# The first step of a fused recurrence and two feed-forward layers: GpSimd takes the k products and the lower weight halves, loads and heads change their order

## The chip, the cores and the metric

The kernel runs on one core of a Trainium2 chip. The metric is the device time of one launch in microseconds (us); the times below are medians of several runs. Five engines work in parallel and wait for each other through semaphores: TensorE (PE in the profile), VectorE (DVE), ScalarE (ACT), GpSimd (POOL) and SyncE (SP), which here only starts transfers.

## The reference

```python
def _attn_ref(r, k, v, w, u):                       # B=4, H=8, S=768, D=48, all float32
    for t in range(S):
        kt, vt, rt, wt = (k[:, :, t], v[:, :, t], r[:, :, t], w[:, :, t])
        cur = np.einsum('bhd,bhe->bhde', u[None] * kt, vt)
        y[:, :, t] = np.einsum('bhd,bhde->bhe', rt, state + cur)
        state = wt[:, :, :, None] * state + np.einsum('bhd,bhe->bhde', kt, vt)

x = y as 3072 tokens x 384
h = x @ w_in;  x = where(h > 0, h, exp(min(h, 0)) - 1) @ w_out          # d_ff 2048
h = x @ w_in2; x = (h / (1 + exp(-1.702 h))) @ w_out2                   # d_ff 2048
```

## The kernel before

The tokens are cut into 8 steps of 384 (half a batch entry). For each step the kernel computes the recurrence of the 8 heads, and it sends the 384 tokens (one group) through the first feed-forward layer while the next step's recurrence runs beside it. After the 8 steps all groups go through the second layer. Every operand of the feed-forward matmuls is split into a high and a low half (`x_hi`, `x_lo`; `w_split` holds both halves of the weights; `g_hi`, `g_lo`), and each product is three matmuls.

The recurrence of a step is chunked. `wtree` holds running products of the decay w over 2, 4, ... 64 tokens ("tree"). In six levels k = 1 to 6, r and k are multiplied by these decays (`update_r`, `update_k`), and after each of them TensorE computes the scores of that distance (`products`); level k+1 waits for its products. `pick_diag` and `pick` take the valid scores out of the banks under a mask (COPY_PREDICATED), `assemble` copies them together, `turn` transposes k, `keys_values` multiplies it with v, `states` runs the chain over the chunks (one copy, then five times `faded = state * wchunk` and `state = faded + psum`), and `outputs` forms y from scores (`from_scores`) and states (`from_state`). Heads lie in two halves of the partitions (`a` = 0, 1) and four slots u; in the first step the slots are worked in two pairs (pair 0: u = 0, 1; pair 1: u = 2, 3), so (k, pair) names a level below, as (2,0).

Two of the 8 heads (slot u = 3) do not fit into the 384 = 3 x 128 rows of x as they come out. Their rows go through the tile `y3` and are moved by transfers of 16 rows into the gaps of `x_raw` ("gap transfers", x_raw<-y). Then `first_split` makes x_hi on ScalarE and x_lo on VectorE, and `up(0, 0, 0)` starts the feed-forward part.

In the first step nothing else is there for TensorE, so its time is bare. The first layer's 16 weight tiles (384 KB each) arrive in it and in the next: `w1_high` on ScalarE makes the high half, `w1_low` on VectorE the lower one, GpSimd starts the transfers (`load`).

From step 1 on TensorE's queue is written out by hand in `step`. `unit(f)` is `up` of tile f+2 (nine matmuls into `hidden`) and `down` of tile f; levels, turns and outputs of the recurrence stand between the units. ScalarE applies the exponential, VectorE `gated`, ScalarE `gate_hi`, VectorE `gate_lo`. The argument s shifts the recurrence behind the units: with s = 1 one whole unit is done before level 1, and `split` of the next group comes after tile 15, with s = 0 after tile 14. Step 1 runs with s = 1, the six steps behind it with s = 0. `near(i+1)`, the first scores of the next step, closes each step.

## Time and profile before

| | |
|---|---|
| median of 3 runs | 1003.53 us (1003.37 to 1005.42) |
| profiled execution: its own time | 1003.23 us |
| its span | 1001.2 us |
| PE busy | 948.9 us, 95% |
| DVE, ACT, POOL busy | 545.1, 456.2, 54.9 us |
| mean granted PE clock | 0.986 of full speed |

The profiled execution took 1003.23 us, of which the span from the first to the last instruction is 1001.2 us. Rows of the timeline and of the chain begin with the start and the length in us from the span's start. A bracket such as [3.17 <-DVE x_lo L730] gives the idle time of the engine just before the row and what ended it. A granted clock of 1.00 is full speed.

### The profile page before, as it was taken

What the parts mean: (1) busy time and instruction counts of PE and PEld (TensorE: products, weight loads), DVE (VectorE), ACT (ScalarE), POOL (GpSimd) and SP (SyncE); (2) the same over time, 40 slices, a digit from 0 to 9 for tenths busy, and PEclk for the clock granted to TensorE, in tenths of its full rate; (3) what the DMA queues carried; (4) which work ended last, traced back from release to release, by engine and by line L of the source; (5) the groups of instructions that cost most, each with busy time, mean ns of one, the idle gap of its engine ahead of it and who ended that gap; (6) DMA issues with size and microseconds to landing.
All of it is one profiled execution on the core that took longest, in us unless ns stands there. A gap on an engine that the chain in (4) does not pass through costs nothing.

```text
span 1001.2 us, 27033 instructions
## 1 busy us (share of the span) xinstructions
PE 948.9 (95%) x11872; PEld 920.2 (92%) x11872; DVE 545.1 (54%) x903; ACT 456.2 (46%) x861; POOL 54.9 (5%) x64
## 2 busy tenths in 40 slices
PE   3659989999999999999999999999999999999998
PEld 3559989989889899999999999999999999999998
DVE  6758757476585686675764444343434343434333
ACT  3344834635536537456455674333333333333332
POOL 3010000000000000000000352000000000000000
PEclk9879999999999999999999999999999999999999
DMA  7242130231211211302102630000000000000000
GB/s 203 73 124 68 41 94 11 49 80 26 56 51 26 55 50 26 102 4 55 49 2 86 252 111 1 1 24 1 24 0 24 0 24 0 24 1 24 1 24 24
DMA packets 15413, 47.29 MB, mean 47 GB/s; under 512 B 2864, under 2 KB 6832, under 8 KB 15312
## 3 DMA queue, kind: packets, MB, share of 16 engines
q1 hardware_dynamic: 12688, 38.19, 13.8%
q0 software_dynamic: 2016, 6.86, 2.3%
q8 instruction: 87, 1.43, 0.6%
q10 hardware_dynamic: 608, 0.70, 0.3%
q14 instruction: 14, 0.11, 0.0%
HBM read 35.71 MB, written 8.85 MB: 45 GB/s over the span
## 4 chain that ended last, share of the span: by engine, by line
PE 91%; issue 3%; DVE 3%; DMA 1%; ACT 1%; POOL 0%; DVEq 0%; ACTq 0%; SPq 0%; POOLq 0%
PE psum L1119 40%; PE psum L1132 39%; PE psum L971 4%; PE psum L1071 2%; PE psum L1032 1%; PE psum L934 1%; PE psum L1066 1%; PE psum L980 1%; PE psum L997 1%; DMA x_raw<-y 1%; DMA arena<-r_channels_dram 1%; DVE arena L641 0%; DVE x_lo L730 0%; DVE blocks L695 0%; ACT x_hi L419 0%
## 5 line engine op out<-in xcount | busy, mean ns | idle before, releaser
L1119 PE MATMUL psum<-x_hi,w_split 128*128 128x384 f32 x1536 | 395.0, 338 | 0.0
L1132 PE MATMUL psum<-g_hi,w_split 128*128 128x384 f32 x1536 | 392.9, 337 | 0.0
L1119 PEld LDWEIGHTS psum<-x_hi,w_split 128*128 128x128 f32 x1536 | 281.3, 189 | 1.4 <-issue 1.4
L1132 PEld LDWEIGHTS psum<-g_hi,w_split 128*128 128x128 f32 x1536 | 278.6, 189 | 0.1
L1119 PE MATMUL psum<-x_lo,w_split 128*128 128x384 f32 x768 | 264.3, 344 | 12.1 <-DVE x_lo L725 5.3
L1132 PE MATMUL psum<-g_lo,w_split 128*128 128x384 f32 x768 | 262.3, 342 | 0.8 <-issue 0.7
L444 ACT ACTIVATE g_hi<-gate 128x384 fp32r<-128x384 f32 x256 | 134.5, 525 | 175.8 <-DVE gate L743 93.5
L748 DVE TENSOR_TENSOR g_lo<-gate,g_hi 128x384 fp32r<-128x384 f32 x256 | 142.7, 557 | 118.9 <-ACT g_hi L444 118.9
L741 DVE TENSOR_TENSOR gate<-expo,psum 128x384 f32<-128x384 f32 x128 | 70.8, 553 | 162.9 <-ACT expo L440 162.9
L1119 PEld LDWEIGHTS psum<-x_lo,w_split 128*128 128x128 f32 x768 | 144.6, 188 | 14.5 <-DVE w_split L769 5.5
L1132 PEld LDWEIGHTS psum<-g_lo,w_split 128*128 128x128 f32 x768 | 145.0, 189 | 3.8 <-issue 1.6
L440 ACT ACTIVATE expo<-psum 128x384 f32<-128x384 f32 x128 | 63.0, 492 | 172.9 <-PE psum L1119 172.9
L743 DVE SCALAR_TENSOR_TENSOR gate<-expo,psum 128x384 f32<-128x384 f32 x128 | 70.9, 554 | 128.4 <-ACT expo L435 128.3
L433 ACT ACTIVATE expo<-psum 128x384 f32<-128x384 f32 x128 | 62.6, 489 | 146.0 <-PE psum L1119 145.7
L635 DVE TENSOR_TENSOR arena<-arena 128x1536 f32<-128x1536 f32 (+1 forms) x54 | 85.1, 1575 | 9.8 <-PE psum L971 8.9
L435 ACT ACTIVATE expo<-expo 128x384 f32<-128x384 f32 x128 | 67.2, 525 | 4.0
L971 PEld LDWEIGHTS psum<-arena 128*32 128x32 f32 (+1 forms) x3840 | 41.9, 112 | 21.3 <-issue 16.7
L971 PE MATMUL psum<-arena 128*32 128x32 f32 (+1 forms) x3840 | 47.5, 204 | 12.8 <-issue 9.1
L641 DVE TENSOR_TENSOR arena<-arena 128x768 f32<-128x768 f32 (+1 forms) x54 | 46.5, 862 | 0.0
L328 POOL DMA_DIRECT2D x_raw<-y x21 | 10.1, 486 | 425.4 <-DVE y L720 425.4
L695 DVE COPY_PREDICATED blocks<-masks,psum 128x384 f32<-128x384 int32 x40 | 30.3, 757 | 2.0 <-DVE blocks L695 1.6
L388 ACT ACTIVATE blocks<-blocks 32x768 f32<-32x768 f32 x32 | 26.9, 840 | 1.2 <-DVE blocks L695 0.6
(75 smaller groups left out, 448.0 us busy)
## 6 DMA issues: line engine op xcount, KB each, us to landing
v_sb<-v_tokens_dram SPq DMA_DIRECT2D x8, 576.0 KB, 5.9
arena<-w_channels_dram SPq DMA_DIRECT2D x14, 288.0 KB, 4.8
arena<-k_channels_dram SPq DMA_DIRECT2D x14, 288.0 KB, 4.4
arena<-r_channels_dram SPq DMA_DIRECT2D x14, 288.0 KB, 4.8
x_scratch<-x_sb SPq DMA_DIRECT2D x7, 576.0 KB, 3.2
arena<-x_scratch SPq DMA_DIRECT2D x1, 4032.0 KB, 12.9
staging<-weights_dram POOLq DMA_DIRECT2D x10, 384.0 KB, 3.6
blocks<-weights_dram SPq DMA_DIRECT2D x9, 384.0 KB, 3.9
```

What stands on the lines that cost most here:

```text
L433: act.activation(expo[:, f % 2, :], hidden(f), ACT.Relu, scale=-1.0).then_inc(neg_done, 1)
L435: act.activation(expo[:, f % 2, :], expo[:, f % 2, :], ACT.Exp, scale=-1.0).then_inc(exp_done, 1)
L440: act.activation(expo[:, f % 2, :], hidden(f), ACT.Sigmoid, scale=1.702).then_inc(exp_done, 1)
L444: act.activation(g_hi[:, f % 4, :], gate[:, f % 2, :], ACT.Copy).then_inc(hi_done, 1)
L635: return dve.tensor_tensor(z, z, by, ALU.mult)
L641: return dve.tensor_tensor(z, z, d[:, :, 1:2].to_broadcast([P, d.shape[1], h]), ALU.mult)
L741: dve.tensor_tensor(gate[:, f % 2, :], expo[:, f % 2, :], hidden(f), ALU.mult).then_inc(gate_done, 1)
L743: dve.scalar_tensor_tensor(out=gate[:, f % 2, :], in0=expo[:, f % 2, :], scalar=-1.0, in1=hidden(f), op0=ALU.add, op1=ALU.max).then_inc(ga ...
L748: dve.tensor_tensor(g_lo[:, f % 4, :], gate[:, f % 2, :], g_hi[:, f % 4, :].bitcast(F32), ALU.subtract).then_inc(lo_done, 1)
L971: mm = pe.matmul(bank[32 * j:32 * j + n, at:at + 32].rearrange("p (a b h) -> p a b h", a=2, h=h), kk[:, u, o:o + n], r[:, :, u, o:o + 32]. ...
L1119: mm = pe.matmul(hidden(f), w_tile(f, lo, m * P), xx, start=n == 0, stop=n == 3 * KT - 1)
L1132: mm = pe.matmul(acc(to, m), w_tile(f, lo, (KT + m) * P), gg, start=f == 0 and n == 0, stop=f == NF - 1 and n == 2)
```

## The change

In the first step:

- SP loads r of a pair ahead of w. ScalarE issues k of pair 1 only after its table load. SP, not GpSimd, starts the first five weight tiles, right behind the first loads.
- VectorE multiplies only r (`grow_r_pair`). GpSimd multiplies k (`grow_k_pair`) and makes the whole tree of pair 1 (`tree_second`). The products wait for both.
- All 16 `w1_low` run on GpSimd. Loads of later tiles stand between them in its queue.
- The clearing of `blocks` moves from GpSimd to VectorE.
- The outputs of slot u = 3 have two banks of their own (`FIRST[6 + c % 2]`) and are computed first (`first_outputs`); `y3` is copied from them by ScalarE and VectorE at once, and the gap transfers (four on SP, two on ScalarE) start before the other outputs are done. The rest of x_raw is copied in pieces of 48 rows, which leave the gaps alone.
- The tree of step 1 comes after `first_split` on VectorE.

In step 1, s goes from 1 to 0, and the weight tiles' high halves take other places in ScalarE's queue (8 and 9 behind tiles 0 and 1, 10 to 15 behind tiles 2 to 7).

```diff
+                def tree_second(m):
+                    us = slice(2, 4)
...
+                    pool.tensor_tensor(dst[:, us], s4[:, :, :, 0], s4[:, :, :, 1], ALU.mult).then_inc(tree_done, 1)
+                def grow_k_pair(k, pair):
...
+                    pool.wait_ge(lev_first[pair], k)
+                    pool.wait_ge(w_first[pair], 32)
...
+                    pool.tensor_tensor(z, z, d[:, :, 1:2].to_broadcast([P, d.shape[1], h]), ALU.mult).then_inc(updk_first[pair], 1)
...
+                def w1_low(f):
+                    pool.wait_ge(whi_done, f + 1)
+                    at = 2 * f * WF
+                    pool.tensor_tensor(w_split[:, at + WF:at + 2 * WF], w1_raw[w1_place(f)],
+                                       w_split[:, at:at + WF].bitcast(F32), ALU.subtract).then_inc(wlo_done, 1)
+                grow_k_pair(1, 0)
+                for m in range(6):
+                    tree_second(m)
+                grow_k_pair(2, 0)
+                grow_k_pair(1, 1)
+                for k in range(3, 7):
+                    grow_k_pair(k, 0)
+                    grow_k_pair(k - 1, 1)
+                grow_k_pair(6, 1)
+                for f in range(NF):
+                    w1_low(f)
+                    if f < 3:
+                        pool.wait_ge(wlo_done, f + 1)
+                        load(f + NW1)
+                    elif 5 <= f < NF - 3:
+                        pool.wait_ge(wlo_done, f + 1)
+                        load(f + 3)
...
+                def first_outputs():
...
+                    for c in (0, 2, 4):
+                        for a in range(2):
+                            from_scores(c, U - 1, a)
+                            mm = from_scores(c + 1, U - 1, a)
+                    mm.then_inc(y3_first, 1)
...
+                    pe.wait_ge(state_done, N_STATE[0])
+                    pe.wait_ge(y3_first, 1)
+                    for c in range(1, NC):
+                        for a in range(2):
+                            mm = from_state(c, U - 1, a)
+                    mm.then_inc(y3_first, 1)
...
-                outputs(0, 0, 0)
+                first_outputs()
                 up(0, 0, 0)
                 near(1)
                 up(0, 0, 1)
-                step(0, 1, 1, 0, 0, s=1)
+                step(0, 1, 1, 0, 0)
```

GpSimd's queue, from its clearing of `arena` on, before:

```order
L317 MEMSET arena 128x768 x4
L318 MEMSET blocks 128x2304
L321 DMA staging<-weights_dram 128x768 x2
L321 DMA x_sb<-weights_dram 128x768
L321 DMA expo<-weights_dram 128x768
L321 DMA gate<-weights_dram 128x768
L321 DMA staging<-weights_dram 128x768 x2
L321 DMA x_sb<-weights_dram 128x768
```

And the same place in the changed kernel (L366 multiplies k, L352 is the tree of pair 1):

```order
L339 MEMSET arena 128x768 x4
L366 ISA
L366 TENSOR_TENSOR arena<-arena 128x384
L352 TENSOR_TENSOR arena<-arena 128x384
L352 TENSOR_TENSOR arena<-arena 128x192
L352 TENSOR_TENSOR arena<-arena 128x96
L352 TENSOR_TENSOR arena<-arena 128x48
L352 TENSOR_TENSOR arena<-arena 128x24
L352 TENSOR_TENSOR wchunk<-arena 128x12
L366 TENSOR_TENSOR arena<-arena 128x192x2
L366 TENSOR_TENSOR arena<-arena 128x384
```

The transfers are gone from the start of this queue; k of (1,0), the six tree products, then k of (2,0) and (1,1) stand there, ten more k products follow, and behind them the 16 lower halves (L382).

VectorE's queue at the end of the first step's levels, before (L676 and L695 are picks, L635 is r, L641 is k, L769 is `w1_low`, L704 to L712 are the states):

```order
L676 COPY_PREDICATED blocks<-masks,psum 128x384 x2
L635 TENSOR_TENSOR arena<-arena 128x2x12x32
L641 TENSOR_TENSOR arena<-arena 128x12x32
L695 COPY_PREDICATED blocks<-masks,psum 128x384
L695 COPY_PREDICATED blocks<-masks,psum 128x192x2
L695 COPY_PREDICATED blocks<-masks,psum 128x96x4
L695 COPY_PREDICATED blocks<-masks,psum 128x48x8
L695 COPY_PREDICATED blocks<-masks,psum 128x24x16
L769 TENSOR_TENSOR w_split<-staging,w_split 128x768 x2
L704 COPY state<-psum 128x192
L709 TENSOR_TENSOR faded<-state,wchunk 128x192
L712 TENSOR_TENSOR state<-faded,psum 128x192
```

And in the changed kernel (L747 and L766 are picks, L707 is r):

```order
L747 COPY_PREDICATED blocks<-masks,psum 128x384 x2
L707 TENSOR_TENSOR arena<-arena 128x2x24x16
L766 COPY_PREDICATED blocks<-masks,psum 128x384
L707 TENSOR_TENSOR arena<-arena 128x2x12x32
L766 COPY_PREDICATED blocks<-masks,psum 128x192x2
L766 COPY_PREDICATED blocks<-masks,psum 128x96x4
L766 COPY_PREDICATED blocks<-masks,psum 128x48x8
L766 COPY_PREDICATED blocks<-masks,psum 128x24x16
L775 COPY state<-psum 128x192
L780 TENSOR_TENSOR faded<-state,wchunk 128x192
L783 TENSOR_TENSOR state<-faded,psum 128x192
```

The first pick now stands ahead of the last r product, the k products and the two lower halves are gone, and the states follow the picks directly.

TensorE's queue around level 1 of step 1, before: the last third of `up` of tile 3, the level, and the start of `down` of tile 1.

```order
L1119 MATMUL psum<-x_lo,w_split 128x384
L1119 MATMUL psum<-x_hi,w_split 128x384 x2
L971 MATMUL psum<-arena 32x32 [waits pick_done,upd_done]
L971 MATMUL psum<-arena 32x32 x47
L1132 MATMUL psum<-g_lo,w_split 128x384 [waits lo_done]
L1132 MATMUL psum<-g_hi,w_split 128x384 x2
```

In the changed kernel the same rows are the last third of `up` of tile 2, the level, and the start of `down` of tile 0.

```order
L1230 MATMUL psum<-x_lo,w_split 128x384
L1230 MATMUL psum<-x_hi,w_split 128x384 x2
L1030 MATMUL psum<-arena 32x32 [waits pick_done,upd_done]
L1030 MATMUL psum<-arena 32x32 x47
L1243 MATMUL psum<-g_lo,w_split 128x384 [waits lo_done]
L1243 MATMUL psum<-g_hi,w_split 128x384 x2
```

The level moved ahead by `down` of tile 0 and `up` of tile 3, 18 matmuls, which now follow it.

## Rows read from the trace of the kernel before

**Rows 1.** The page, part 2: busy tenths of TensorE in 40 slices of 25 us

```profile
PE   3659989999999999999999999999999999999998
```

**Rows 2.** Windows: span; length; busy (count) PE, PEld, DVE, ACT, POOL; clock; DMA; GB/s

```profile
65.00:137.40 72.40, 63.86 (x989) 60.37 (x987) 51.22 (x78) 41.11 (x76) 4.68 (x9) 0.93 0.29 75
142.90:205.40 62.50, 61.17 (x989) 57.92 (x987) 41.73 (x69) 34.11 (x66) 1.43 (x3) 1.00 0.21 52
80.00:127.80 47.80, 47.27 (x825) 44.98 (x824) 37.09 (x60) 30.41 (x57) 4.15 (x8) 1.00 0.22 58
127.80:137.40 9.60, 6.43 (x30) 5.71 (x28) 3.55 (x5) 4.13 (x7) 0.00 (x0) 0.82 0.57 130
```

**Rows 3.** Timeline, 6 to 13 us: the first waits for loads

```profile
6.07 1.10 ACT L364 ACTIVATE arena<-arena,ucol 128x384 f32<-128x384 f32 x2
7.04 1.70 DVE L622 TENSOR_TENSOR arena<-arena 128x384 f32<-128x384 f32 x5 [1.87 <-DMA arena<-w_channels_dram]
...
9.65 1.51 PE L934 MATMUL psum<-arena 128*32 128x64 f32 x48 [9.65 <-DMA arena<-r_channels_dram]
...
11.65 1.25 POOL L321 DMA_DIRECT2D staging<-weights_dram  x2 [6.18 <-DMA arena<-w_channels_dram]
11.85 0.96 DVE L635 TENSOR_TENSOR arena<-arena 128x768 f32<-128x768 f32 x1 [2.90 <-PE psum L971]
```

**Rows 4.** Timeline, 15 to 46 us, VectorE: levels, picks, lower halves, states

```profile
15.92 0.55 DVE L641 TENSOR_TENSOR arena<-arena 128x384 f32<-128x384 f32 x1
...
28.77 0.96 DVE L635 TENSOR_TENSOR arena<-arena 128x768 f32<-128x768 f32 x1 [0.26 <-PE psum L980]
...
38.67 0.59 DVE L695 COPY_PREDICATED blocks<-masks,psum 128x384 f32<-128x384 int32 x1 [0.26 <-DVE blocks L695]
39.14 1.83 DVE L769 TENSOR_TENSOR w_split<-staging,w_split 128x768 fp32r<-128x768 f32 x2
40.87 0.36 DVE L704 COPY state<-psum 128x192 f32<-128x192 f32 x1
...
44.85 0.36 DVE L712 TENSOR_TENSOR state<-faded,psum 128x192 f32<-128x192 f32 x1
```

**Rows 5.** The chain that ended last, from the outputs to the first `up`

```profile
49.51 0.56 DVE x_raw L719
...
50.99 2.50 DMA x_raw<-y
53.51 0.53 ACT x_hi L414
...
54.77 3.22 PE psum L1119 x9
```

**Rows 6.** The same chain around level 1 of step 1

```profile
69.65 2.09 issue
71.74 1.14 PE psum L971 x66
72.87 2.75 issue
```

**Rows 7.** Timeline, TensorE: first matmul behind the split of group 1 and of group 2

```profile
132.50 0.44 PE L1119 MATMUL psum<-x_lo,w_split 128*128 128x384 f32 x1 [3.17 <-DVE x_lo L730]
...
202.08 0.44 PE L1119 MATMUL psum<-x_lo,w_split 128*128 128x384 f32 x1 [0.54 <-DVE x_lo L730]
```

**Rows 8.** Timeline, 569 to 577 us: GpSimd and VectorE side by side

```profile
569.52 1.85 POOL L349 TENSOR_TENSOR w_split<-blocks,w_split 128x768 fp32r<-128x768 f32 x1 [1.28 <-ACT w_split L463]
572.93 1.36 DVE L735 TENSOR_TENSOR x_lo<-arena,x_hi 128x1152 fp32r<-128x1152 f32 x1 [0.50 <-ACT x_hi L427]
573.71 2.29 POOL L349 TENSOR_TENSOR w_split<-blocks,w_split 128x768 fp32r<-128x768 f32 x1 [2.35 <-ACT w_split L463]
575.74 0.67 DVE L748 TENSOR_TENSOR g_lo<-gate,g_hi 128x384 fp32r<-128x384 f32 x1 [0.59 <-ACT g_hi L444]
```

**Rows 9.** The page, part 5: g_lo in all groups (busy, mean ns, idle before)

```profile
L748 DVE TENSOR_TENSOR g_lo<-gate,g_hi 128x384 fp32r<-128x384 f32 x256 | 142.7, 557 | 118.9 <-ACT g_hi L444 118.9
```

**Rows 10.** Timeline, SP: two gap transfers of the first step

```profile
50.34 1.23 SPq L243 DMA_DIRECT2D x_raw<-y  x2
```

More of the change, by code:

```diff
@@ L148, in build @@
         level_open, pick_open, gap_open = sem("level_open"), sem("pick_open"), sem("gap_open")
-        w1_in = [sem(f"w1_in{q}") for q in range(NW1)]
+        w1_in = [sem(f"w1_in{q}") for q in range(3)]
         w2_in = [sem(f"w2_in{q}") for q in range(NW2)]
@@ L195, in tokens, with y3_first_view, x_first_rows @@
             return chunks[:, z, 0:2] if z < 2 else chunks[:, :, 2]
+        def y3_first_view(par):
+            return (y3[:].rearrange("p m (c two t) -> p two c m t", c=NB, two=2)[:, par],
+                    FIRST[6 + par][:, 0:NB * CH].rearrange("p (c m t) -> p c m t", c=NB, m=1))
+        def x_first_rows(z, a):
+            rows = slice(64 * a, 64 * a + D)
+            return tokens(x_raw[:], z)[rows], of_heads(0, z, 0, KT)[rows]
         def of_heads(i, z, u0, u1):
@@ L278, in _ @@
                                      r_dram[0, a][:, cols]).then_inc(r_first[pair], 16)
+                    sp.wait_ge(cleared_w, pair + 1)
+                    first_pair(arena[:, 3 * UT:4 * UT], w_dram, pair, w_first)
                 sp.dma_start(v_sb[:].rearrange("p c u a e -> p (c u a e)"), v_dram[0]).then_inc(v_in, 16)
                 sp.dma_start(ident[:, :], ident_dram).then_inc(ident_in, 16)
+                for f in range(NW1):
+                    sp.dma_start(w1_raw[f], weights1[f]).then_inc(w1_first[f], 16)
                 step(0)
@@ L542, in _, with load_k @@
                 act.dma_start(ucol[:, :], ucol_dram).then_inc(ucol_in, 16)
-                for pair in range(2):
+                def load_k(pair):
                     act.wait_ge(cleared_k, pair + 1)
@@ L556, in _ @@
                     w1_high(f)
-                for z in range(3):
-                    kt_copy(0, z)
                 act.wait_ge(cleared_b, 1)
@@ L576, in _ @@
                 act.wait_ge(wlo_done, NW1)
-                for f in range(2):
-                    whole(0, f)
+                whole(0, 0)
                 w1_high(8)
-                step(1, 0, 0, s=1)
+                whole(0, 1)
+                w1_high(9)
+                step(1, 0, 0)
                 with act.Fori(1, B - 1) as b:
@@ L786, in step @@
                     grow_k(i, 2)
-                    lower(8)
                     pick(i, 1)
@@ L794, in step @@
                     gate_lo(g, 4 + s)
-                    lower(9)
                     pick(i, 4)
@@ L808, in step @@
                     gate_lo(g, 7 + s)
-                    lower(12)
                     pick(i, 16)
@@ L1209, in _ @@
                 up(0, 0, 1)
-                step(0, 1, 1, 0, 0, s=1)
+                step(0, 1, 1, 0, 0)
                 with pe.Fori(1, B - 1) as b:
```

218 lines of the change are left out of this document (134 added, 84 removed).

## The prediction, made before the change was run

> **What bounds the kernel now.** I read the busy slices first [rows 1]: TensorE is at 8 or 9 tenths from the fourth slice on, and at 3 to 6 tenths in the first three. The change touches nothing behind step 1, so only the first 140 us can give anything. Then the windows [rows 2]. From the `up` of tile 2 to the first scores of the next step (`near`), step 1 takes 72.4 us and step 2 takes 62.5 us, for the same 989 recorded matmuls. So the first step is bare waiting, and step 1 carries 9.9 us that its successor doesn't. Between 80 and 127.8 us TensorE is busy for 47.27 of 47.8 us: work taken off other engines there is worth nothing. The chain shows the rest: r's load holds the first scores until 9.65 [rows 3], VectorE runs the levels and picks until 39.26 and the states until 45.21 [rows 4], the gap transfers hold x_hi until 53.51 [rows 5], and TensorE waits 2.09 and 2.75 us around level 1 [rows 6] and 3.17 us behind the split [rows 7]. (Each of these ends is the row's start and length together.)
>
> **What GpSimd and VectorE do to each other.** This decides the case, and the trace has two encounters [rows 8]. A GpSimd product of 768 columns takes 1.85 us alone. One that starts at 573.71, while VectorE's x_lo (two inputs in SBUF) runs until 574.29, takes 2.29 us and ends at 576.00, which is 1.71 us after x_lo's end. VectorE's g_lo, started at 575.74 under it, takes 0.67 us instead of the usual 0.56 [rows 9], and ends 0.41 us after 576.00. Both fit one reading: of two such instructions only one reads at a time, and about 0.15 us of each (1.85 less 1.71, 0.56 less 0.41) lies outside that hold. I take it. A GpSimd product then holds VectorE's two-input products for 1.71 us at 768 columns, or 2.23 ns a column. VectorE's own holds are 0.96 - 0.15 = 0.81 us for r and less for the others.
>
> The Trainium skill says the same, and it is what speaks against this change: "SBUF — State Buffer", section "SBUF: two separate sides", has the port pair that the two share as an exclusive lock for the whole instruction, between a GpSimd operation and a VectorE operation with two SBUF inputs. By that rule the sum is the one below; by free sharing it would be the first rival's.
>
> **The change, part by part.**
>
> *Start.* r of pair 0 moves from fourth to second in the line of loads, w from second to third. w arrived second at 7.04 [rows 3], so r should be there by then, and the two k scalings (1.10 us [rows 3]) end near 7.2, as k is in by 6.07 or earlier. First scores at about 7.2 instead of 9.65: the first r product at 9.4 instead of 11.85, -2.4 us.
>
> *Tree on GpSimd.* w of pair 1 is now last of six loads. Fifth of six it freed GpSimd at 11.65 [rows 3]; I put it at 12.5. The six tree products have 756 columns: 756 x 2.23 ns + 6 x 0.15 = 2.6 us, with waits on its own semaphore 2.9. Two r products of VectorE (0.8 each) fall into it, and half a microsecond is lost ahead of it. k of (2,0) has 384 columns: 384 x 2.23 ns + 0.15 = 1.0 us. It stands behind the tree and ends near 12.5 + 0.6 + 2.9 + 0.8 + 1.0 = 17.8 us. Before it ended at 16.47 [rows 4]. The head start is gone: +1.3 us.
>
> *Levels.* VectorE needed 0.96 + 0.55 us for a pair of r and k, less overlap. Now r holds 0.81 and k 0.86 us, in turn: 1.67 a pair, 3.3 a level. Before, from k of (2,0) at 15.92 to r of (6,0) at 28.77 [rows 4], four levels took 12.85 us, 3.2 each, since VectorE also waited for TensorE. The pace is the same, and with one round trip less at the end r of (6,0) starts near 28.8 again. No gain from the split.
>
> *Picks.* From r of (6,0) to the last pick took 10.5 us (28.77 to 39.26 [rows 4]). Three k products go (some 0.4 us each), the first pick moves into a wait for TensorE, but r and k of (6,1) queue for the hold. I take 9.3: picks end at 38.1, -1.2 us.
>
> *States.* They no longer stand behind two lower halves (1.83 us [rows 4]) and start near 38.4 instead of 40.87. But GpSimd, which ends its last k near 35.5, now runs lower halves one behind the other, 1.86 us each, and five of the chain's eleven links (`faded`) read two SBUF tiles. Before the chain took 4.3 us (40.87 to 45.21). If every `faded` meets a lower half it takes 11.5, if the transfers that GpSimd issues between its products let most through, 7.3. I take 9.2, as three such gaps exist for five links: the states end at 47.6 instead of 45.21, +2.4 us.
>
> *y and the gaps.* From the states' end to the first `up` took 54.77 - 45.21 = 9.6 us [rows 4, 5]. The gap transfers now start about 1 us after the states: three issues of 0.6 us on SP [rows 10] ahead of the fourth, and its landing of 2.5 us [rows 5], make 5.3 with it. The rest of y takes 4.4 us on TensorE (45.21 to 49.51 before, and one wait more), and then come three copies of 0.56 [rows 5] on VectorE instead of the transfers: 6.1 us. So x_hi starts at +6.1 instead of +8.3 (53.51 - 45.21), -2.2. Then 1.26 us to the first matmul as before. The lower half of tile 7 is started just then, since its high half stands right ahead of x_hi on ScalarE, and holds the first x_lo: +1.0 us. First `up` at 47.6 + 6.1 + 1.26 + 1.0 = 56.0 against 54.77: +1.2 us in all for the first step.
>
> *Step 1.* Before, 82.6 us lie between the first `up` (54.77) and `near(2)` (137.4), 10.2 of them ahead of tile 2's `up` (at 65.0), 72.4 behind. With s = 0 the latter part is arranged as in step 2, which takes 62.5 [rows 2]. TensorE still waits for level 1's k product. Two lower halves (1.9 us) leave VectorE's line ahead of it, a hold of 1.71 us may come into it, and the level now stands one `down` and one `up` nearer; the tree fits into the time of `near`. I keep 2.1 us [rows 6]. What goes is the 3.17 us behind the split, as step 2's 0.54 shows [rows 7], with the low clock behind it (granted 0.82 in that stretch, 1.00 in step 2's [rows 2]), some 1.5 us. The 2.75 us inside level 1 [rows 6] wait for nothing that the profile shows; its place moves by 18 matmuls, so it may go or stay. I put clock after the wait and this at 1.7 us. The lower halves leave VectorE (8 x 0.95 us), but each holds it for 1.71 us; between levels 2 and 3 VectorE has no slack: +0.8 us. Sum: 10.2 + 62.5 + 2.1 + 1.7 + 0.8 = 77.3 against 82.6, -5.3 us.
>
> *Total.* +1.2 - 5.3 = -4.1 us. Against the profiled execution's own 1003.23 us (0.3 below the median of the runs shown) that is 999.1 us. Most of it is the step from s = 1 to 0, not the work given to GpSimd.
>
> **Bounds.** The hold: between nothing and every link met, the states end between 43 and 50. The k product on GpSimd: not below its share of columns, 0.93 us, nor above a whole 1.85. The wait inside level 1: 0 to 2.75. w of pair 1: 11.65 to 13.5.
>
> **Rivals.**
>
> *No hold, the engines share.* Two encounters may be chance. Then the tree ends at 15.5, a level takes 3.0 us (TensorE's own round trip and its own pauses), the states and the scores' matmuls end at 42.3, and the first `up` comes 7.4 us later, at 49.7 instead of 54.77 (6.1 + 1.26 as above) and level 1 isn't held either: -5.1 - 5.3 - 1.6 = -12.0, 991.2 us (1.6: level 1's product and levels 2 and 3 without a hold). Chance 0.13.
>
> *The k product is dearer on GpSimd, and it ends slower.* Its inputs are strided and one is broadcast; no row shows such a form. Eleven of them stand in one line. At 1.0 us they keep pace; each tenth more costs 1.1 us. From 1.37 us on the 4.1 us are gone, and at 1.55 the kernel is 2 us slower: 999.1 + 11 x 0.55 = 1005.2. For it speaks that the 1.85 us is the only price known, against it that a column costs VectorE the same in both forms. Chance 0.11.
>
> *The lower halves hold VectorE back in step 1.* VectorE is busy for 37.1 of 47.8 us there [rows 2]; 8 x 0.95 go and up to 8 x 1.71 us of hold come. If the levels come late by 1 us each, four of them, the 4.1 us are lost: 1003.2, no change. Against it: TensorE's queue has one unit of slack for all but the levels, and a lower half starts behind g_lo, when VectorE's next product has begun. Chance 0.13.
>
> **How the numbers follow.** The forecast, 999.1, has 0.63; its own range is 996 to 1002.5, from the states' end (45.7 to 50) and the wait inside level 1. 0.2% is 2 us, about what a measurement can tell: faster is below 1001.5, slower above 1005.5. Faster: 0.56 of the forecast's 0.63 and all of the first rival's 0.13, 0.69. Slower: 0.08 from the second and 0.02 from the third, 0.10. Same: 0.21. The range, 992 to 1004, leaves out most of the first rival and the slower part of the second, about 2 in 10.
>
> **What would show it.** The k products on GpSimd at 1.0 us alone and near 1.8 when r runs; `faded` at up to 2 us each instead of 0.36; k of (2,0) ended near 17.8; the first `up` near 56; step 1's wait behind the split down to under 1 us at full clock. It is wrong if `faded` stays at 0.36 beside lower halves (then it is 991), if k products take over 1.4 us, or if TensorE waits more than a microsecond in all between 80 and 125 us.

## The result and the profile after

The changed kernel takes 1011.18 us (median of 6 runs, 1008.21 to 1012.43), the kernel before beside it 1004.93 (6 runs, 1003.37 to 1006.34): ratio 1.0064, 95% interval 1.0048 to 1.0080. It is 0.6% slower. The prediction had 999.1 us, a range of 992 to 1004 and a chance of 0.10 for slower. The profiled execution took 1011.4 us (span 1009.4).

The page's busy tenths, TensorE's to set beside [rows 1]: its second slice is at 5, where it was at 6, and GpSimd is busy in the first five. TensorE's granted clock (third row) is lowest in the second slice, where it waits most.

```profile
PE   3559999999999899999999999999999999999998
...
POOL 6836100000000000000000262000000000000000
PEclk8569999999999999999999999999999999999999
```

Timeline of the start, of VectorE and GpSimd, beside [rows 3]:

```profile
9.14 0.56 DVE L694 TENSOR_TENSOR arena<-arena 128x384 f32<-128x384 f32 x1 [1.52 <-DMA arena<-w_channels_dram]
9.73 1.21 DVE L694 TENSOR_TENSOR arena<-arena 128x192 f32<-128x192 f32 x1
10.87 0.94 DVE L707 TENSOR_TENSOR arena<-arena 128x768 f32<-128x768 f32 x1
```
```profile
9.26 1.47 POOL L366 TENSOR_TENSOR arena<-arena 128x384 f32<-128x384 f32 x1 [5.74 <-PE psum L1030]
12.34 0.83 POOL L352 TENSOR_TENSOR arena<-arena 128x384 f32<-128x384 f32 x1 [1.61 <-DMA arena<-w_channels_dram]
...
15.75 1.01 POOL L366 TENSOR_TENSOR arena<-arena 128x384 f32<-128x384 f32 x1
```

The first scores now start at 6.98, but w of pair 0, behind k and r, comes at 9.14 instead of 7.04, and the second tree product (9.73, 1.21 us for 0.36) stands behind GpSimd's k of (1,0). So the first r product comes at 10.87 (11.85 before), not at 9.4. k of (2,0) on GpSimd ends at 16.76, but TensorE, which stopped at 14.43 among the first products of pair 1, goes on with them and with level 2 only at 17.43:

```profile
17.43 0.82 PE L1030 MATMUL psum<-arena 128*32 128x32 f32 x67 [3.00 <-issue]
```

The 3.00 us ahead of them wait for nothing that the profile shows.

The states start at 41.19, later than the last pick (it ends at 39.99). The chain that ended last shows what they waited for:

```profile
35.24 1.62 POOL arena L366
...
36.91 1.54 PE psum L1056 x6
...
39.18 1.99 PE psum L1091 x64
...
41.19 0.37 DVE state L775
```

The last k product, k of (6,1), runs on GpSimd until 36.86; the turns (L1056) and keys times values (L1091) follow, and then the first copy of the states. Before, VectorE ended that product at 34.56. So it is GpSimd's line, not VectorE's picks, that lets the states start here.

The timeline of VectorE and GpSimd while the states run, to set beside the last lines of [rows 4]. The states are a chain of eleven operations, here called links. L780 is the link `faded`, a product of two SBUF tiles; L783 adds from PSUM; L369 issues a weight transfer, L382 is a lower half of a weight tile:

```profile
41.85 0.56 POOL L369 DMA_DIRECT2D staging<-weights_dram  x1 [0.31 <-POOL w_split L382]
...
42.37 2.10 DVE L780 TENSOR_TENSOR faded<-state,wchunk 128x192 f32<-128x192 f32 x1
42.43 1.81 POOL L382 TENSOR_TENSOR w_split<-x_sb,w_split 128x768 fp32r<-128x768 f32 x1
...
44.51 0.35 DVE L783 TENSOR_TENSOR state<-faded,psum 128x192 f32<-128x192 f32 x1
44.54 0.56 POOL L369 DMA_DIRECT2D x_sb<-weights_dram  x1 [0.30 <-POOL w_split L382]
44.89 5.78 DVE L780 TENSOR_TENSOR faded<-state,wchunk 128x192 f32<-128x192 f32 x1
45.12 1.82 POOL L382 TENSOR_TENSOR w_split<-expo,w_split 128x768 fp32r<-128x768 f32 x1
...
46.91 1.79 POOL L382 TENSOR_TENSOR w_split<-gate,w_split 128x768 fp32r<-128x768 f32 x1
48.66 1.79 POOL L382 TENSOR_TENSOR w_split<-staging,w_split 128x768 fp32r<-128x768 f32 x1
50.71 0.35 DVE L783 TENSOR_TENSOR state<-faded,psum 128x192 f32<-128x192 f32 x1
50.75 0.56 POOL L369 DMA_DIRECT2D staging<-weights_dram  x1 [0.30 <-POOL w_split L382]
51.16 2.20 DVE L780 TENSOR_TENSOR faded<-state,wchunk 128x192 f32<-128x192 f32 x1
```

A link that takes 0.36 us alone takes 5.78: it starts at 44.89, during the issue at 44.54 and before the half of 45.12, and ends after the third half, at 50.67. The additions from PSUM stay at 0.35. From 41.19 to 54.53 the chain takes 13.3 us, where it took 4.3.

The chain that ended last, beside [rows 5]: x_hi, x_lo, the first `up`.

```profile
60.44 0.53 ACT x_hi L474
60.99 1.51 DVE x_lo L796
...
62.63 3.22 PE psum L1230 x9
```

The first `up` is 7.9 us later than before (54.77). Step 1 gives most of it back: `near(2)` starts at 138.84 against 137.38. But another 6.6 us go behind it, between `near(2)` and `near(7)`: 347.8 us (138.84 to 486.66) against 341.3 (137.38 to 478.64). Together these are 8.0 of the 8.2 us between the two profiled executions. The starts of `near` of the steps 2 to 7 are from TensorE's timeline at its line; from one to the next (steps 2 to 6) it takes 67.9, 71.1, 72.3, 69.1, 67.4 us after, and 68.0, 68.5, 70.0, 67.3, 67.4 before.

### The profile page after: what moved, and what is told of

Its sections match the earlier page's. It is cut to its first block, busy times and chain, and to the rows that moved or that the text cites. A ratio compares the mean times of both kernels' runs of the same rounds, so it can differ in the third digit from the quotient of the medians.

```text
span 1009.4 us, 27078 instructions
## 1 busy us (share of the span) xinstructions
PE 951.9 (94%) x11872; PEld 922.3 (91%) x11872; DVE 550.2 (55%) x872; ACT 456.9 (45%) x861; POOL 104.4 (10%) x90
## 4 chain that ended last, share of the span: by engine, by line
PE 91%; issue 3%; DVE 2%; DMA 1%; POOL 1%; ACT 0%; SPq 0%; DVEq 0%; POOLq 0%; ACTq 0%
PE psum L1230 40%; PE psum L1243 39%; PE psum L1030 3%; PE psum L1130 2%; PE psum L1091 1%; PE psum L1039 1%; PE psum L1125 1%; DVE faded L780 1%; PE psum L1056 1%; PE psum L991 1%; DMA x_raw<-y 1%; DMA arena<-w_channels_dram 1%; POOL arena L366 0%; PE psum L1179 0%; POOL arena L352 0%
## 5 line engine op out<-in xcount | busy, mean ns | idle before, releaser
L819 DVE TENSOR_TENSOR g_lo<-gate,g_hi 128x384 fp32r<-128x384 f32 x256 | 147.7, 577 | 117.8 <-ACT g_hi L504 117.7
L707 DVE TENSOR_TENSOR arena<-arena 128x1536 f32<-128x1536 f32 (+1 forms) x54 | 89.4, 1658 | 12.2 <-PE psum L1030 10.7
L495 ACT ACTIVATE expo<-expo 128x384 f32<-128x384 f32 x128 | 67.2, 525 | 4.0
L713 DVE TENSOR_TENSOR arena<-arena 128x768 f32<-128x768 f32 x42 | 41.3, 984 | 0.0
L766 DVE COPY_PREDICATED blocks<-masks,psum 128x384 f32<-128x384 int32 x40 | 30.3, 757 | 2.2 <-DVE blocks L766 1.8
```

Source lines behind the costliest of these rows:

```text
L495: act.activation(expo[:, f % 2, :], expo[:, f % 2, :], ACT.Exp, scale=-1.0).then_inc(exp_done, 1)
L707: return dve.tensor_tensor(z, z, by, ALU.mult)
L713: return dve.tensor_tensor(z, z, d[:, :, 1:2].to_broadcast([P, d.shape[1], h]), ALU.mult)
L819: dve.tensor_tensor(g_lo[:, f % 4, :], gate[:, f % 2, :], g_hi[:, f % 4, :].bitcast(F32), ALU.subtract).then_inc(lo_done, 1)
```

## The experiments

Fifteen kernels ran; ratios are to the kernel before on the same chip. "First `up`" is the start of the first `up` matmul. A "half" is a lower or higher half of a weight tile. Times inside a kernel are from its one profiled execution.

**e1_s0: the kernel before with the step order s = 0 alone.**

```diff
-                step(0, 1, 1, 0, 0, s=1)
+                step(0, 1, 1, 0, 0)
```


> The kernel before with only step 1's s changed from 1 to 0 (and the six high halves placed accordingly). The first step is as before. My account of the change: from the first up to near(2) it takes 77 us instead of 82.6, because the 3.17 us wait behind the split and the low clock after it go, so 5 us less: 998 to 1000. Rival: the gain is given back behind step 1, in the loop, as in the changed kernel, whose near(2) came only 1.4 us later than before's but whose near(7) came 8.1 us later: then near(2) comes 5 us earlier and the end 0 to 2 us earlier.

Measured: 1000.51 us, ratio 0.9954 (0.9939 to 0.9969). First `up` at 53.3, `near(2)` at 131.2: 77.9 us between them, for 82.6 before and 77.3 predicted. The gain between them, 4.7 us, is near the 5.3 predicted for this part of the change, and the step order alone beats both kernels. The rival falls: `near(2)` to `near(7)` takes 341.5 us, as before. The first `up` is 1.5 us earlier than before (54.8) though nothing ahead of it changed, and 1.2 us earlier (53.6) in e2 below: by so much two executions of the same first step differ, and a smaller difference in one start shows nothing by itself.

**e2_pad8: the kernel before with eight empty instructions at the start of TensorE's program.** There TensorE waits for its loads anyway. The changed kernel's part ahead of the loop has eight instructions more too, 1375 for 1367.

```diff
+                for _ in range(8):
+                    pe.sem_inc(level_open, 1)
                 pe.wait_ge(cleared_p, 3)
```


> The kernel before with eight empty semaphore increments at the start of TensorE's queue, where it waits for the first loads. The changed kernel has eight instructions more in front of the loop than before has (1375 against 1367). Theory A, the place of the loop's code decides its pauses: near(2) comes as before, and near(2) to near(7) takes 346 to 348 us instead of 341.2, the whole 4 to 6 us longer. Theory B, the place does nothing: within 0.5 us of before everywhere, and the 6.7 us of the changed kernel behind step 1 have another cause.

Measured: 1008.34 us, ratio 1.0038 (1.0017 to 1.0060). The steps take 67.6, 70.8, 70.3, 69.1, 67.4 us: as in the changed kernel, the second loses 2.3 us and the fourth 1.8. `near(2)` comes at 138.3, 0.9 late, and from there to `near(7)` it takes 345.2 us, 3.9 more than before (theory A had 346 to 348 and stands; B falls). Eight more instructions ahead of the loop cost time in it, without any work changed.

**e3_late_low: the changed kernel with GpSimd's halves held until the states are done.**

```diff
                 grow_k_pair(6, 1)
+                pool.wait_ge(state_done, N_STATE[0])
```


> The changed kernel with GpSimd's lower halves held back until the states are done. Theory, the hold: the eleven links of the states take 4.3 us instead of 13.3, so near 45.5 instead of 54.5, the first up comes 8 to 9 us earlier, at 54 to 55 (some 1 us of hold by the first lower halves may come back), and near(2) 6 to 9 us earlier: 1003 to 1005. Rival: the states are slow for another reason (TensorE's own matmuls or the banks), and they still take over 10 us; or the first up then waits for the lower half of tile 0, which starts at 45.5 and ends at 47.4, which is early enough.

Measured: 1010.7 us, ratio 1.0054 (1.0037 to 1.0071). The states take 4.3 us again (40.79 to 45.14): the halves alone stretched them. But the load of tile 5 now waits for half 0, ScalarE waited 7.11 us for it in front of its copy of y3, and the first `up` came at 59.8, not at 54 to 55: the total misses the 1003 to 1005 expected.

**e4_probe: GpSimd's products measured behind the end of the kernel before.**


> The kernel before with a probe behind its end (the output is untouched). GpSimd: three plain products of 384 columns, three in the form of the k product (h = 1, 4, 32), then four of 768 columns back to back beside six VectorE products of 192 columns with two SBUF inputs, then four of 768 beside six VectorE sums with one input in SBUF and one in PSUM. My price: 1.0 us for each 384-column product in every form. Rival: the broadcast form is dearer, 1.4 us or more. Hold: the sums with PSUM take 0.36 us each beside GpSimd; of the products with two SBUF inputs, one that meets GpSimd's row of four waits until the whole row is done (5 us or more) if GpSimd keeps the hold from one instruction to the next, and at most 1.8 us if it gives it up between them.

Measured: a plain product of 384 columns starts every 0.95 us (0.99 us long); in the k products' form 1.16 us at h = 1, 0.91 at h = 4, 0.84 at h = 32. Products of 768 columns beside VectorE's of two SBUF inputs alternate, one to one: VectorE's start every 1.88 us. With the second input in PSUM VectorE's take 0.34 us. The second rival of the prediction (k dearer than 1.0 us by itself) falls, and so does the reading that a link waits for several halves whenever they stand in a row.

**e5_all_dve: the changed kernel with k, tree and halves all on VectorE.** And **e6_low_dve**, the halves alone.

```diff
-                grow_k_pair(1, 0)
...
+                    update_k(0, k, slice(2 * pair, 2 * pair + 2)).then_inc(updk_first[pair], 1)
...
+                    lower(9)
                     pick(i, 4)
```


> The changed kernel with the k products, the tree of pair 1 and all lower weight halves back on VectorE, at the kernel before's places; load order, y3 first, the late tree and the single step order stay. Theory (GpSimd's work costs VectorE more than it takes off it): the picks end near 39 to 40 us as in both kernels, the states take 4.3 us instead of 13.3, and the first up projection starts at 50 to 52 us (before 54.8, after 62.6), since the y3-first order and the late tree then act alone; near(2) at 127 to 130 us, total 995 to 1000 us. Rival (the move of loads, the y3 banks or the late tree cost the time, not GpSimd): states and first up projection stay late, over 58 us, total over 1006.

> The changed kernel with only the lower weight halves back on VectorE; GpSimd keeps the k products and the tree of pair 1. Theory (the halves beside the states are what cost the start): states 4.3 us, first up projection 51 to 53 us, near(2) 127 to 131, total 995 to 1001, about level with the version with everything on VectorE, because the levels end at 39 to 40 us either way. Rival (the k products cost as much as the halves): the total stays above 1004.

Measured: 1020.91 us, ratio 1.0159 (1.0111 to 1.0206), and 1021.71, ratio 1.0179 (1.0128 to 1.0231). Neither theory nor rival said this. The start is as the theory had it: the states take 4.3 us and the first `up` comes at 53.2 and 53.6. But in e5 step 1 then takes 97.1 us to `near(2)` at 150.3. ScalarE's higher halves in it:

```profile
87.31 0.84 ACT L482 ACTIVATE w_split<-staging 128x768 fp32r<-128x768 f32 x1 [5.14 <-DMA staging<-weights_dram]
...
97.29 0.84 ACT L482 ACTIVATE w_split<-x_sb 128x768 fp32r<-128x768 f32 x1 [7.05 <-DMA x_sb<-weights_dram]
```

The buffers are three deep. A load waits for the lower half of three tiles before; that stands late in VectorE's line, and ScalarE's next higher half waits for the load, with the gating behind it: ScalarE waited 5 to 7 us for a load in four of the eight halves of step 1. The changed kernel's order of higher halves works only with GpSimd's early lower halves. e6 shows the same (6.04 us ahead of such a half at 89.50). Moving an engine's work "back" alone had made a new wait.

**e7_late_low2: e3, with ScalarE's higher halves 5 to 7 moved behind its part of the bonus.**

```diff
+                pool.wait_ge(state_done, N_STATE[0])
...
                 act.wait_ge(wlo_done, NW1)
+                w1_high(5)
+                w1_high(6)
                 whole(0, 0)
+                w1_high(7)
```


> The changed kernel with GpSimd's lower halves held until the states are done, and ScalarE's higher halves 5 to 7 moved behind its part of the bonus, so that no load stands ahead of its copies. Theory (the 13.3 us of the states are GpSimd's hold alone): states 4.3 us, first up projection near 55 us, near(2) 132 to 135, as the halves now stand beside the x split and the tree of VectorE instead; total 1000 to 1006. Rival (the y path is late for another reason): first up projection over 58 us although the states take 4.3.

Measured: 1006.21 us, ratio 1.0025 (1.0009 to 1.0040); first `up` at 57.3, `near(2)` at 136.1. The states take 4.3 us, so that the theory stands, though the first `up` is 2 us later than its 55. The halves now stand beside the split: the first x_lo, issued at 53.33, took 3.87 us (0.55 alone), through the halves of 53.20 and 54.98. A second wait through two in a row, where e4 had them alternate.

**e8_probe2 and e12_probe3: which form of product waits through several?**


> Kernel before with four trials behind its end, in each of which GpSimd makes four products of 768 columns, one behind the other (1.8 us each), released together with VectorE's work of 192 columns: trial 0 one plain product of two SBUF inputs, trial 1 one with its second input broadcast as the faded links have it, trial 2 the links' chain (broadcast product, addition from PSUM, twice, each behind a semaphore), trial 3 the same chain with plain products. Theory A (VectorE gets its turn at the next border between GpSimd's products): no VectorE product of two SBUF inputs takes over 2.2 us. Theory B (a broadcast or dependent product loses several turns, as the faded link of 5.78 us did): trials 1 or 2 show a VectorE product of 3.6 us or more, trial 0 and 3 do not (broadcast) or 3 does too (dependence).

> Kernel before with four trials behind its end, each four GpSimd operations of 768 columns back to back beside VectorE's chain of eight (broadcast product of two SBUF inputs, addition from PSUM, each behind a semaphore). GpSimd's operations are lower halves without and with a satisfied wait ahead of each (trials 0 and 1), then plain products with and without it (trials 2 and 3). Theory A (the lower halves' form keeps VectorE out over several operations): trials 0 and 1 show a VectorE product of 3.6 us or more, trials 2 and 3 none over 2.2. Theory B (the satisfied wait does): 1 and 2 show it, 0 and 3 don't. Theory C (where VectorE's request falls in time decides): no clean split by trial.

Measured: none of them. (Trials 0 and 1 of e8 say nothing: VectorE's product there had begun before GpSimd's.) Over plain, broadcast and dependent products of VectorE, and products and lower halves of GpSimd, with and without a satisfied wait ahead of each, the longest took 1.48 us. Theory A of e8 holds; A and B of e12 fall. C, the moment of VectorE's request, stays open. One held product of e12 and the half that it waited for:

```profile
1007.17 1.48 DVE L958 TENSOR_TENSOR arena<-arena 128x192 f32<-128x192 f32 x1
```
```profile
1006.44 2.00 POOL L365 TENSOR_TENSOR w_split<-staging,w_split 128x768 fp32r<-128x768 f32 x1 [0.53 <-DVE arena L954]
```

What the long waits in the kernels have and the probes lack: a weight transfer that GpSimd issued right ahead of the halves (44.54 in the changed kernel, 52.62 in e7).

**e9_merge: the changed kernel, TensorE's part ahead of the loop at 1367 instructions again.** One semaphore for the r and the k update of a level takes ten waits out, two empty instructions are put in.

```diff
-                    pe.wait_ge(updr_first[pair], k)
-                    pe.wait_ge(updk_first[pair], k)
+                    pe.wait_ge(upd_first[pair], 2 * k)
```


> The changed kernel with the two semaphores of a level's r and k update made into one, which takes ten waits out of TensorE's program, and two empty instructions put at its start, so that its part ahead of the loop has 1367 instructions as in the kernel before, where the changed kernel has 1375. Nothing else moves. Theory (the place of TensorE's code costs what is lost behind step 1, as eight empty instructions showed): the steps behind near(2) take 68.0, 68.5, 70, 67.3 and 67.4 us again instead of 67.9, 71.1, 72.3, 69.1 and 67.5, near(2) stays at 139, total 1003 to 1006. Rival (the change disturbs the later steps otherwise): total 1009 to 1012.

Measured: 1006.63 us, ratio 1.0021 (1.0007 to 1.0036). Windows of the changed kernel's steps 3 and 4, then e9's (columns as in [rows 2]):

```profile
206.70:277.80 71.10, 68.42 (x1197) 64.28 (x1196) 45.41 (x73) 35.77 (x69) 1.44 (x3) 0.98 0.20 46
277.80:350.10 72.30, 67.31 (x1197) 63.45 (x1196) 45.82 (x74) 35.76 (x69) 1.44 (x3) 1.00 0.19 45
```
```profile
208.00:275.40 67.40, 66.64 (x1200) 62.88 (x1199) 45.39 (x73) 35.78 (x69) 1.44 (x3) 1.00 0.20 49
275.40:346.80 71.40, 67.32 (x1197) 63.48 (x1196) 45.74 (x74) 35.75 (x69) 1.44 (x3) 1.00 0.20 46
```

The same matmuls, VectorE and ScalarE work in shorter steps: `near(2)` to `near(7)` is 342.5 us, 5.3 less, and the ratio falls by 0.0043 (4.3 us). The theory stands, though step 4 takes 71.4 us, step 5 68.3, `near(2)` comes at 140.1 and the total is just over 1006. What is left over the kernel before, 2 us, lies ahead of `near(2)`, which is 2.7 us late.

The traces of all thirteen kernels but the probes, those described below among them, divide by this count, whatever else the kernels do. With 1367 instructions ahead of the loop (before, e1, e9, e10, e11, e14, e15) step 3 takes 67.4 to 68.5 us, step 5 67.2 to 68.3 and `near(2)` to `near(7)` 341.3 to 342.5. With 1375 (changed kernel, e2, e3, e5, e6, e7) they take 69.0 to 71.1, 69.0 to 69.5 and 343.4 to 347.8. The changed kernel's trace is the longest of the six: in its step 3 (and e2's) the granted clock was 0.98 and TensorE was busy for 68.4 us, for 66.5 to 67.0 at 1.00 in the others. The 1.8 us that its step 5 takes longer than before are pauses in which TensorE waits for nothing that the profile shows (columns: us in total, times, longest; window 350 to 419 us):

```profile
PE psum L1243 <- issue: 1.1, 1, 1.1
PE psum L1230 <- issue: 0.6, 1, 0.6
```

The start holds such a pause too, ahead of level 2. In the kernels with the changed kernel's order of loads it is 2.73 to 3.77 us with 1375 instructions (changed kernel, e3, e5, e6, e7) and 1.24 to 1.97 with 1367 (e9, e10, e11, e14, e15).

**e10_gate: e9 with halves 0 and 1 at once, 2 to 5 behind the states, 6 and on behind the late tree.**

```diff
+                    if f == 2:
+                        pool.wait_ge(state_done, N_STATE[0])
+                    elif f == 6:
+                        pool.wait_ge(tree_done, 2 * N_TREE)
                     w1_low(f)
```


> The kernel of e9_merge with GpSimd's lower halves 0 and 1 at once, 2 to 5 behind the states, 6 and later behind the late tree, and ScalarE's higher half 6 behind its copy of y3. Theory (the halves cost the start through VectorE's waits alone): states 4.3 to 6 us and done by 46, first up projection at 53 to 55 us, steps behind it as in e9_merge, near(2) at 129 to 132, total 994 to 998. Rival (the halves only cost elsewhere): first up projection over 57 us, total over 1000.

Measured: 998.35 us, ratio 0.9935 (0.9912 to 0.9958); states done at 44.82, first `up` at 54.6, `near(2)` at 133.1 (somewhat later than the 129 to 132 expected). All the changed kernel's work is still on GpSimd; its time is chosen, and ScalarE's higher half 6 comes behind its copy of y3. Together that is 8.6 us under e9.

**e11_y3: the changed kernel's loads, y3 order, late tree and s = 0, with k, tree and halves on VectorE, ScalarE's higher halves as before, 1367 instructions.**

```diff
-                        after = {2: 10, 3: 11, 4: 12, 5: 13, 6: 14, 7: 15}
+                        after = {2: 9, 3: 10, 5: 11, 7: 12, 8: 13, 9: 14, 10: 15}
```


> The changed kernel with the k products, the tree of pair 1 and all lower halves on VectorE, and ScalarE's higher halves in the kernel before's order, with TensorE's part ahead of the loop at 1367 instructions. What is left of the change: load order, y3 first, late tree, single step order. Theory (the round trips of the weight ring made e5's step 1 long, and y3 first gives little): up to near(2) 77 to 78 us, first up projection 53 us, total 998 to 1002, level with the kernel before with the single step order alone (1000.5). Rival (the y3 order is worth its 3 us of hidden transfer): total 994 to 997.

Measured: 994.95 us, ratio 0.9910 (0.9887 to 0.9932), the fastest version. First `up` at 51.9, `near(2)` at 127.8. The theory (y3 first gives little) falls and the rival's total holds: under e1's 0.9954 it is 4.4 us, and the intervals don't meet. But the 4.4 us belong to load order, y3 first and late tree together; no run parts them. Of the 3.4 us by which `near(2)` is earlier than e1's, 1.4 are there at the first `up` and 2.0 come in step 1.

**e13_probe4: products with a transfer issue ahead of them.**

```diff
+                        if (trial, z) in ((1, 0), (2, 2), (3, 0)):
+                            pool.dma_start(w1_raw[0], weights1[trial]).then_inc(probe_q, 16)
+                            if trial == 3:
+                                pool.wait_ge(probe_q, 48)
```


> Kernel before with four trials behind its end: four GpSimd products of 768 columns beside VectorE's chain of twelve (broadcast product, PSUM addition). Trial 0 has no transfer issue, trial 1 one right ahead of the first product, trial 2 one ahead of the third, trial 3 one ahead of the first and a wait for the transfer between. Theory (products that follow a transfer issue without a wait that holds are not left until GpSimd pauses): trial 0 and 3 show waits of one product (1.5 to 2 us), trial 1 one wait through all four products (about 7 us) and trial 2 one through two (about 3.6 us). Rival (the issue doesn't matter): all waits 1.4 to 2.0 us.

Measured, VectorE's timeline: a held product of trial 0, the one of trial 1, and trial 2's last.

```profile
1000.44 1.45 DVE L956 TENSOR_TENSOR arena<-arena 128x192 f32<-128x192 f32 x1
...
1009.99 7.40 DVE L956 TENSOR_TENSOR arena<-arena 128x192 f32<-128x192 f32 x1
...
1025.95 3.70 DVE L956 TENSOR_TENSOR arena<-arena 128x192 f32<-128x192 f32 x1
```

And GpSimd's:

```profile
1009.48 0.61 POOL L360 DMA_DIRECT2D staging<-weights_dram  x1 [2.17 <-DVE arena L952]
1010.10 7.07 POOL L364 TENSOR_TENSOR arena<-arena 128x768 f32<-128x768 f32 x4
```
```profile
1025.26 0.58 POOL L360 DMA_DIRECT2D staging<-weights_dram  x1
1025.87 1.81 POOL L364 TENSOR_TENSOR arena<-arena 128x768 f32<-128x768 f32 x1
1027.62 1.80 POOL L364 TENSOR_TENSOR arena<-arena 128x768 f32<-128x768 f32 x1
```

Without the issue one product is waited for; with it all that follow, 7.40 us through four and 3.70 through two. In both, and in the kernels' long waits (44.89 and e7's 53.33), VectorE's product was asked for during the issue or at most 0.13 us after the next GpSimd product began; whether a later request waits as long, no run shows. In trial 3 VectorE's chain had ended before GpSimd's products began, so it says nothing of the wait between.

**e15_loads_after: e9 with the first three transfers issued behind half 4, and ScalarE's higher halves 5 and 6 behind its copy of y3.**

```diff
-                    if f < 3:
-                        pool.wait_ge(wlo_done, f + 1)
-                        load(f + NW1)
+                    if f == 4:
+                        pool.wait_ge(wlo_done, 3)
+                        for n in range(3):
+                            load(n + NW1)
```


> The kernel of e9_merge with the three weight transfers that GpSimd issues behind halves 0, 1 and 2 all issued behind half 4, and ScalarE's higher halves 5 and 6 behind its copy of y3. Theory (a transfer issue makes VectorE lose its turns): no link of the states takes over 2.3 us, five halves of 1.85 us let one link through each, and the states end 2 to 4 us earlier than in e9_merge (53.7), at 50 to 52. Rival (three halves in a row do it by themselves): one link takes 5 us or more.

Measured: 1001.68 us, ratio 0.9971 (0.9956 to 0.9986), 5.0 us under e9. The links beside five halves in a row, on VectorE's timeline:

```profile
40.33 1.50 DVE L780 TENSOR_TENSOR faded<-state,wchunk 128x192 f32<-128x192 f32 x1
41.86 0.35 DVE L783 TENSOR_TENSOR state<-faded,psum 128x192 f32<-128x192 f32 x1
42.25 1.50 DVE L780 TENSOR_TENSOR faded<-state,wchunk 128x192 f32<-128x192 f32 x1
...
44.24 1.43 DVE L780 TENSOR_TENSOR faded<-state,wchunk 128x192 f32<-128x192 f32 x1
```

Five halves in a row beside the same links, and no wait over 1.50 us: the states end at 46.83 (e9: 53.70), better than the 50 to 52 expected. In e9 three in a row, behind an issue, had held one link for 5.78 us. Halves 5 and 6, which ran beside the states in e9, come only at 49.94 and 52.62 here, since their higher halves moved; so the 5.0 us are the worth of both edits together. That the long waits are the issue's doing is shown by e13.

**e14_k_pool: e11 with the k products and pair 1's tree on GpSimd.** Its diff against e11 is that of e5 and e6 against each other.


> The kernel of e11_y3 with the k products and the tree of pair 1 on GpSimd, so that it is the changed kernel with the lower halves on VectorE in the kernel before's places. Theory (GpSimd's k products hold VectorE's r products about as long as they take off it): first up projection within 1 us of e11_y3's 51.8, total 994 to 997, not to be told from e11_y3. Rival (prediction: the move of k gains 1.2 us): first up projection 1 us earlier and total 993 to 994; the other rival, GpSimd's k costs over 1 us: total over 997.

Measured: 996.21 us, ratio 0.9919 (0.9899 to 0.9939), not to be told from e11. First `up` at 53.6, 1.7 us later: more than the theory's 1 us. VectorE's tree and r products, of e14 and then of e11:

```profile
9.47 1.80 DVE L693 TENSOR_TENSOR arena<-arena 128x384 f32<-128x384 f32 x2 [1.85 <-DMA arena<-w_channels_dram]
11.19 0.95 DVE L706 TENSOR_TENSOR arena<-arena 128x768 f32<-128x768 f32 x1
...
29.75 0.96 DVE L706 TENSOR_TENSOR arena<-arena 128x768 f32<-128x768 f32 x1 [0.78 <-PE psum L1064]
```
```profile
9.04 0.95 DVE L658 TENSOR_TENSOR arena<-arena 128x384 f32<-128x384 f32 x2 [1.42 <-DMA arena<-w_channels_dram]
9.91 0.95 DVE L671 TENSOR_TENSOR arena<-arena 128x768 f32<-128x768 f32 x1
...
28.32 0.96 DVE L671 TENSOR_TENSOR arena<-arena 128x768 f32<-128x768 f32 x1 [0.26 <-PE psum L1032]
```

From the r product of (1,0) to that of (6,0) both take the same, 18.6 and 18.4 us, though VectorE makes the k products in e11 alone. Of the 1.7 us, 1.3 are lost ahead of that: w came 0.4 us later, and k of (1,0) on GpSimd holds the second tree product, 0.9 us. All of it is near what two executions differ by (e1).

## Why the prediction was wrong

- *The hold.* Right as a mechanism: VectorE's products of two SBUF inputs wait for GpSimd's, PSUM forms don't (e4, e13). The Trainium skill has this as an exclusive lock for a whole instruction ("SBUF — State Buffer", section "SBUF: two separate sides"). The trace agrees: a VectorE product that takes 0.36 us alone takes 1.45 beside GpSimd products of 1.8 (e13, trial 0).
- *States: the first step that failed.* The prediction said 9.2 us, 7.3 "if the transfers that GpSimd issues between its products let most through", 11.5 "if every `faded` meets a lower half". Measured: 13.3, over its upper bound, which took a link to wait for one half at most. The sign of the transfers was wrong: VectorE doesn't get through at an issue, it loses its turns in all that follows without a pause (5.78 us here, 7.40 in e13). With the three issues behind the halves no link waits over 1.50 us (e15).
- *Start, levels, picks.* Picks predicted to end at 38.1 and the states to start at 38.4; measured 39.99 and 41.19. "r should be there by then" held (first scores at 6.98), but w came 2.1 us later than before and k of (1,0) held the tree: the first r product 1.5 us late. "The pace is the same" held (e14 beside e11); TensorE's pause of 3.00 us ahead of level 2 was not in the sum; with 1367 instructions it is 1.24 to 1.97 us, so 1 to 1.8 us of it go with the code's place as well. So r of (6,0) stood at 30.32, not 28.8. The path was wrong, too: the sum had the states behind the picks, with 0.3 us between. They waited 1.2 us for keys times values, which waited for the turns of the last k product; this ended at 36.86 on GpSimd, not "near 35.5".
- *Tree on GpSimd.* Start 12.34 (12.5 predicted), k of (2,0) ended at 16.76 (17.8): a little better.
- *y and the gaps.* x_hi 5.9 us behind the states (6.1 predicted, 8.3 before); x_lo's hold 1.0 us as predicted. Right. First `up` at 62.63, not 56.0: of the 6.6 us, 4.1 are the longer chain and 2.8 its later start, less 0.3 behind it.
- *Step 1.* 76.2 us (77.3 predicted), no wait behind the split, and none that the trace puts down to one of GpSimd's halves in it. Right, and e1 shows that it is the step order that gives it. The rival of the halves in step 1 falls. One sign that the prediction had set itself did come: TensorE waits 1.6 us in all between 80 and 125 us (0.5 before), but in pauses without a cause in the profile.
- *"The change touches nothing behind step 1": the second step that failed.* 6.7 us went there, though no instruction in those steps changed. The term stood at nothing, without a row for it. Eight empty instructions alone cost 3.8 us (e2), taking the eight out gives 4.3 back (e9), and all thirteen traces divide by the count. The 342.5 us of e9 for 341.3 before lie within what kernels with 1367 instructions differ by. What the eight instructions do is not shown; that it is the fetching of TensorE's code stays a guess. The Trainium skill ("Runtime: NRT & Kernel Launch", section "Instruction fetch mechanics") has code fetched in blocks of 256 instructions, the crossing of a block mostly hidden, and a taken branch to a block outside the two at hand as a stall. No run here shows a fetch; that the loss moves with the count would fit.

In sum, from the predicted 999.1: +6.6 for the first `up`, -1.1 for step 1, +6.8 behind it: 1011.4, the profiled execution (+6.8 for 6.7, as the predicted `near(2)` and total are rounded). Its 6.8 are partly chance: the median of the changed kernel is only 4.3 us over e9's. The forecast had the hold right and the kernel's step order right; it had one cost beside the hold with the wrong sign, and one at nothing. What the change was worth in parts, by ratios to the kernel before: s = 0 alone -4.6 us; with loads, y3 order and late tree -9.0 (e11); k and tree on GpSimd no gain (e14, -8.1); the halves on GpSimd as the change has them, with ScalarE's order of higher halves, +10.2 (e9 less e14), held back behind the states +1.6 (e10 less e14, inside their intervals); the code's place +4.3 (changed kernel less e9).

## What to carry over

Work moved to GpSimd isn't free for VectorE: where it stands beside a dependent chain of two-input SBUF products it must be timed (holding the halves until the chain is done gave 8.6 us, with the other moves of e10), and it paid to issue transfers from GpSimd behind a run of its products, not right ahead of it. Before a saving of a few us is credited to a change, count how many instructions it adds ahead of the loop of the engine that bounds the kernel, and try the kernel before with as many empty ones. When a part is undone to test it, see which buffers its place kept free: e5 and e6 came out 16 to 18 us slower than the kernel before by a weight round trip, and said little of what they were made for.

## What the runs showed of the hardware

- GpSimd's and VectorE's products of two SBUF inputs alternate one to one when both stand in line (a VectorE product of 0.36 us takes 1.45 beside 1.8 us ones). A VectorE product that is asked for while GpSimd issues a transfer, or just after, waits until GpSimd pauses instead: 7.40 us for four products, 3.70 for two (e13), 5.78 for three halves (changed kernel, and 5.78 again in e9).
- GpSimd's product of 384 columns takes 0.84 to 1.16 us with a broadcast input, by the length of the runs it is broadcast over, and 0.99 plain (e4).
- Eight empty instructions ahead of a loop of 1610, under a wait that hides them, cost 3.8 us (e2, ratio 1.0017 to 1.0060).
